# The last 64 channels of the centred rows transposed two tiles at a time in a fused convolution, Fourier and MLP kernel

## The reference

```python
batch, seq, d_model = (4, 4224, 192)          # H = 8 heads, K = 7 taps, rank 32, F = 768

# 1: causal depthwise convolution with softmaxed taps
x_unf = x_pad[:, idx, :].reshape(B, S, K, H, group)
x = np.einsum('hk,bskhg->bshg', w, x_unf).reshape(B, S, D)
# 2: low rank mixing over the sequence and the first MLP
u = x + ((x.transpose(0, 2, 1) @ U) @ V).transpose(0, 2, 1)
x = u + np.maximum(u @ w_ch1, 0.0) @ w_ch2
# 3: Fourier mixing over sequence and channels, normalisation, the second MLP
mixed = np.real(np.fft.fft(np.fft.fft(x, axis=1), axis=2))
u = x + mixed
mu = np.mean(u, axis=-1, keepdims=True)
var = np.mean((u - mu) ** 2, axis=-1, keepdims=True)
un = (u - mu) / np.sqrt(var + 1e-06)
out = u + np.maximum(un @ w2_ch1, 0.0) @ w2_ch2
```

## Time and profile before

| what | value |
|---|---|
| device time, median of 3 runs | 1253.76 us (1250.06 to 1254.5) |
| device time of the profiled execution | 1252.18 us |
| its span, first to last instruction | 1250.4 us |
| PE busy | 1218.8 us, 97% of the span |
| PEld busy | 1193.4 us, 95% |
| DVE busy | 821.1 us, 66% |
| ACT busy | 646.3 us, 52% |
| POOL busy | 425.8 us, 34% |
| mean granted clock of TensorE | 0.994 of full speed |

### The profile page before, as it was taken

How to read it: one execution, slowest core, us unless ns; L and a number is a source line. 1 busy time by engine, 2 the same in 40 slices (tenths; PEclk the granted TensorE clock), 3 DMA queues, 4 the chain that set the end, 5 groups by cost and what they waited for, 6 DMA issues and landing times.

```text
span 1250.4 us, 23662 instructions
## 1 busy us (share of the span) xinstructions
PE 1218.8 (97%) x8448; PEld 1193.4 (95%) x8448; DVE 821.1 (66%) x2191; ACT 646.3 (52%) x1603; POOL 425.8 (34%) x542
## 2 busy tenths in 40 slices
PE   6799999999999999999999999999999999999998
PEld 5699999999998999999999999999999999999998
DVE  4555576787765577655557777765666877766654
ACT  5355555444466555445555555544445555554553
POOL 0123352343344254333333244421212344533331
PEclk9899999999999999999999999999999999999999
DMA  8957553244556532224434322222323232322220
GB/s 283 279 185 232 178 160 91 85 147 141 163 168 216 196 123 90 74 69 135 136 96 138 115 92 87 92 70 81 95 86 106 85 101 92 92 93 86 86 68 29
DMA packets 87677, 154.46 MB, mean 124 GB/s; under 512 B 11448, under 2 KB 46627, under 8 KB 87516
## 3 DMA queue, kind: packets, MB, share of 16 engines
q1 hardware_dynamic: 79944, 133.95, 34.0%
q0 software_dynamic: 7616, 18.99, 4.7%
HBM read 94.59 MB, written 63.32 MB: 126 GB/s over the span
## 4 chain that ended last, share of the span: by engine, by line
PE 93%; DVE 2%; DMA 2%; issue 1%; POOL 1%; ACT 1%; SPq 0%; POOLq 0%; ACTq 0%
PE bank L802 20%; PE bank L803 9%; PE bank L783 8%; PE bank L790 7%; PE bank L791 7%; PE bank L787 7%; PE bank L784 7%; PE bank L839 4%; PE bank L806 4%; PE bank L892 4%; PE bank L855 2%; PE bank L915 2%; PE bank L857 2%; PE bank L856 2%; PE bank L876 2%; PE bank L805 2%
## 5 line engine op out<-in xcount | busy, mean ns | idle before, releaser
L987 ACT ACTIVATE ht<-bank 128x384 fp32r<-128x384 f32 x528 | 259.4, 491 | 506.8 <-PE bank L791 501.2
L1170 DVE SCALAR_TENSOR_TENSOR ht<-bank,ht 128x384 fp32r<-128x384 f32 x528 | 293.5, 556 | 339.6 <-ACT ht L987 332.6
L802 PE MATMUL bank<-w,ht 128*128 128x384 f32 x1320 | 418.6, 366 | 0.8 <-DVE ub L1178 0.5
L803 PE MATMUL bank<-w,ht 128*128 128x192 f32 x1320 | 331.0, 251 | 0.0
L1417 POOL TENSOR_TENSOR ub<-ub,tmp 128x576 f32<-128x576 f32 x88 | 126.0, 1432 | 462.5 <-DVE ub L1178 312.6
L802 PEld LDWEIGHTS bank<-w,ht 128*128 128x128 f32 x1320 | 248.8, 188 | 4.0 <-issue 3.1
L803 PEld LDWEIGHTS bank<-w,ht 128*128 128x128 f32 x1320 | 252.4, 191 | 0.0
L783 PE MATMUL bank<-uth,w1h 128*128 128x384 f32 x528 | 189.1, 358 | 0.0
L787 PE MATMUL bank<-utl,w1h 128*128 128x384 f32 x528 | 178.6, 338 | 0.3 <-DVE utl L1195 0.2
L790 PE MATMUL bank<-uts,w1s 128*128 128x384 f32 x528 | 178.5, 338 | 0.3
L784 PE MATMUL bank<-uth,w1l 128*128 128x384 f32 x528 | 178.2, 337 | 0.0
(11 more groups left out here) (118 smaller groups left out, 2218.8 us busy)
## 6 DMA issues: line engine op xcount, KB each, us to landing
f1t<-f_copy SPq DMA_DIRECT2D x44, 396.0 KB
ub<-x_two SPq DMA_DIRECT2D x44, 288.0 KB
mix<-mixed SPq DMA_DIRECT2D x44, 288.0 KB, 3.3
out<-ub SPq DMA_DIRECT2D x44, 288.0 KB
xin<-in_x SPq DMA_DIRECT2D x12, 864.0 KB, 6.9
x_conv<-xin SPq DMA_DIRECT2D x12, 756.0 KB
vch<-v_split SPq DMA_DIRECT2D x42, 192.0 KB
mixed<-rowk SPq DMA_DIRECT2D x88, 74.2 KB
```

What stands on the lines that cost most here:

```text
L802: e.matmul(dn[t][:, 0:2 * D], hh, w2[ph][:, m, :], start=(m == 0), stop=False)
L803: mm = e.matmul(dn[t][:, 0:D], hl, w2[ph][:, m, 0:D], start=False, stop=False)
L987: e.activation(hth[q % 4], up[q % 3][:, 0:TOK], ACT.Relu).then_inc(act_h, 1)
L1170: e.scalar_tensor_tensor(htl[q % 4], up[q % 3][:, 0:TOK], 0.0, hth[q % 4].bitcast(F32), ALU.max, ALU.subtract).then_inc(dve_l, 1)
```

## The change

In the second phase only, `un` is split into `un_first` (128 channels of each tile) and `un_rest` (the last 64 channels of the three tiles side by side, 192 columns). `centre` writes `un_first` in slot 4 with three activations of 128 columns, and a new `centre_rest` writes `un_rest` in slot 5 with three activations of 64 columns. `turn_centred` makes three transposes of `un_first`, one transpose of 128 columns of `un_rest` (tiles 0 and 1 together: their channels come out in partitions 0 to 63 and 64 to 127), and one of the last 64 columns (tile 2). ACT copies the second bank in two activations, DVE makes the low parts in two operations. For the middle tile the high part then lies in partitions 64 to 127 of `uts` and the low part in 0 to 63. The semaphore `act_un` counts six per block instead of three. The first phase is as it was.

```diff
-        un = sb("un", [128, TB, D], F32)
+        un_first = sb("un_first", [128, TB, 128], F32)
+        un_rest = sb("un_rest", [128, TB * 64], F32)
...
+        def outer_tiles(t, par, p0):
+            return t[p0:p0 + 64, par].rearrange("p (t q) -> p t q", t=TB)[:, 0::2, :]
...
+            def turn_centred(n):
+                k = count(n)
+                o, q = empty(e, ("turn", n, 0))
+                for t in range(TB):
+                    e.wait_ge(act_un, k * TB * 2 + t + 1)
+                    mm = e.transpose(o[:, t * 128:(t + 1) * 128], un_first[:, t, :], ident[:])
+                mm.then_inc(pe_tb[q], 1)
+                o, q = empty(e, ("turn", n, 1))
+                e.wait_ge(act_un, (k + 1) * TB * 2)
+                e.transpose(o[:, 0:128], un_rest[:, 0:128], ident[:])
+                e.transpose(o[0:64, 128:256], un_rest[:, 128:192], ident[:]).then_inc(pe_tb[q], 1)
...
-                copy(uts[0:64, par], o[0:64, 0:TOK]).then_inc(act_tb[q], 1)
+                if phase(n) == 0:
+                    copy(uts[0:64, par], o[0:64, 0:TOK]).then_inc(act_tb[q], 1)
+                else:
+                    copy(outer_tiles(uts, par, 0), o[0:64, 0:256].rearrange("p (t q) -> p t q", t=2))
+                    copy(uts[64:128, par, 128:256], o[64:128, 0:128]).then_inc(act_tb[q], 1)
...
-                    e.activation(un[:, t, :], u_slot(n)[:, t, :], ACT.Identity, bias=nm[:, n % 2, t:t + 1]).then_inc(act_un, 1)
+                    e.activation(un_first[:, t, :], u_slot(n)[:, t, 0:128], ACT.Identity, bias=nm[:, n % 2, t:t + 1])\
+                        .then_inc(act_un, 1)
+
+            def centre_rest(n):
+                for t in range(TB):
+                    e.activation(un_rest[:, t * 64:(t + 1) * 64], u_slot(n)[:, t, 128:D], ACT.Identity,
+                                 bias=nm[:, n % 2, t:t + 1]).then_inc(act_un, 1)
...
                     if m == 4 and ahead(n, 2) is not None:
                         deviation(n + 2)
                         centre(n + 2)
+                    if m == 5 and ahead(n, 2) is not None:
+                        centre_rest(n + 2)
...
-                e.tensor_tensor(uts[64:128, par], o[0:64, 0:TOK], uts[0:64, par].bitcast(F32), ALU.subtract)\
-                    .then_inc(tb_free[q], 1)
+                if phase(n) == 0:
+                    e.tensor_tensor(uts[64:128, par], o[0:64, 0:TOK], uts[0:64, par].bitcast(F32), ALU.subtract)\
+                        .then_inc(tb_free[q], 1)
+                else:
+                    e.tensor_tensor(outer_tiles(uts, par, 64), o[0:64, 0:256].rearrange("p (t q) -> p t q", t=2),
+                                    outer_tiles(uts, par, 0).bitcast(F32), ALU.subtract)
+                    e.tensor_tensor(uts[0:64, par, 128:256], o[64:128, 0:128], uts[64:128, par, 128:256].bitcast(F32),
+                                    ALU.subtract).then_inc(tb_free[q], 1)
```

More of the change, by code:

```diff
@@ L827, in turn @@
             def turn(n):
[L828 to L832, removed]
+                if phase(n) == 1:
+                    return turn_centred(n)
+                taken(e, ("low", n, 0))
+                taken(e, ("low", n, 1))
                 for half in range(2):
@@ L836, in turn @@
                     for t in range(TB):
-                        if ph == 1 and half == 0:
-                            e.wait_ge(act_un, k * TB + t + 1)
-                        mm = e.transpose(o[0:m, t * 128:(t + 1) * 128], src[:, t, c], ident[:])
+                        mm = e.transpose(o[0:m, t * 128:(t + 1) * 128], u_slot(n)[:, t, c], ident[:])
                     mm.then_inc(pe_tb[q], 1)
+            def turn_centred(n):
[9 more added lines that the diff above has]
+                e.transpose(o[0:64, 128:256], un_rest[:, 128:192], ident[:]).then_inc(pe_tb[q], 1)
             def dft128(n):
```

## The result

| | median us | runs | profiled execution us | its span us |
|---|---|---|---|---|
| before | 1252.96 (1250.06 to 1254.5) | 5 | 1252.18 | 1250.4 |
| changed | 1260.84 (1259.79 to 1261.95) | 5 | 1261.35 | 1259.4 |

The ratio of the times is 1.0062, with a 95% interval of 1.0050 to 1.0074: the changed kernel is 7.9 us slower. The forecast was 1257.4 us in a range of 1250 to 1263. So the sign was right, and the loss about twice the 3.6 us that were forecast.

A forecast was written before the change was run, and what follows sets the result against it. PE was taken to bound the kernel, with 93% of the chain. Terms -4.8 + 6.4 + 0.8 + 0.6 + 0.6 = +3.6 us gave a span of 1254.0 and a forecast median of 1257.4 us, range 1250 to 1263.

The forecast's parts named there:

- the transposes: PE at the turn: one step of 0.11 us goes per block, 44 x 0.11 = 4.8 us saved.
- The rival of whole transposes: At the turn on PE, the full 0.27 us is saved per block, 12.0 us instead of 4.8: 1250.2 us, chance 0.03.
- the twelve boundaries: Boundaries without groups or convolution: PE has no slack and waits 0.53 us at each, 12 x 0.53 = 6.4 us lost.
- The price of a piece: ACT at the block's end: 64-column activations cost 0.24 us each, three 0.72 us (bounds 0.57 and 1.04).
- the rival of dear pieces: Between L987 and L998 on ACT, three small pieces cost 0.35 us each: +8.9 us, 1262.7 us, chance 0.20.
- The cover at boundaries with groups: At the other 28 boundaries group_rows holds DVE or PE has more work: nothing lost, 0.3 us to spare with groups.
- the forecast's three terms for the 16 boundaries' waits: PE waits 0.53 us at twelve boundaries, 0.42 after blocks 42 and 64, 0.30 after 44 and 66: 6.4, 0.8, 0.6.
- blocks 44 and 66: First use of the turned rows there: PE already waits, so 0.14 us plus 0.15 for the split, 0.6 us for both.
- pure gain: At the block boundaries the pieces are absorbed and the transpose step goes: -4.8 us, 1249.0 us, chance 0.12.
- No price, except in blocks 44 and 66: Split copy and subtraction at the turn: 1.0 us of cover before uts' low part is read, so no cost elsewhere.
- under cover: Work behind partial on ACT (L987, some 0.3 us late) and on DVE is used two slots later, so costs nothing.
- the split's 0.15 us on DVE: At the turn, one more subtraction costs DVE 0.15 us fixed time; ACT's extra copy about as much.

The follow-up runs named there:

- the pieces alone: Kernel before with only the centre split, its three 64-column activations in slot 5, six transposes and single copies: 1261.42 us, ratio 1.0062.
- the pieces in slot 0 and the mean last: Changed kernel with centre_rest in slot 0 of the next block and DVE's aggregate and less_mean at the end of slot 2: 1246.54 us, ratio 0.9943.
- the pieces in slot 0: Changed kernel with centre_rest moved from slot 5 to slot 0 of the next block, behind hidden: 1251.77 us, ratio 0.9986.
- Moving the mean out of the way: DVE's aggregate and less_mean moved behind turned_low and x2_low: 1251.61 us in the changed kernel (single execution), 1250.44 us in the kernel before.

## Why the prediction was right, and where it fell short

**Right: the transposes.** One step of 0.11 us goes, not a length of 0.27: the turns without groups go from 11.16 to 11.04 or 11.05 us wherever the pieces are out of the way. The rival of whole transposes is out.

**Right: the twelve boundaries.** Their term was 12 x 0.53 - 12 x 0.11 = 5.0 us, and the stretch is 5.1 us longer. The price of a piece (0.24 us a step) was right too, so the rival of dear pieces is out although the time came near it; that was by another path. The cover at boundaries with groups held as well: with the pieces alone those blocks are as long as before, to 0.06 us. Between slot 5 and slot 0 the pieces cost 7.7 us by the stretches with six transposes (8.0 - 0.3) and 9.0 with five (7.05 + 1.96); the forecast's three terms for the 16 boundaries' waits were 6.4 + 0.8 + 0.6 = 7.8. Of these the 0.30 us after blocks 44 and 66 measured 0.23, and the 0.42 after blocks 42 and 64 0.47.

**Right: blocks 44 and 66**, the steps at the first use (0.29 us of 0.3), by the forecast's own working: with the pieces alone, where PE and the chain are late by the same, nothing is added there. **Right: pure gain is out**, at the places that the change chose; with the pieces in slot 0 and the mean last, most of it is there (3.8 us of 4.8).

**The step that failed** is "No price, except in blocks 44 and 66" for the split at the turn, together with the 44 x 0.11 that went before it and with the work behind `partial` that was to be "under cover". I read the cover of the turned rows, 1.0 us, at one block without groups and without `dft128`, and carried it to all. The stretches are 3.5 us longer than the forecast's terms, and the blocks say where:

- In blocks 26 to 31, 46, 47 and 68 to 74 `group_out` stands behind `turned_low` for its bank, and the 0.11 us are hardly gained: the turns go from 13.62 to 13.59, not to 13.51. That is 1.2 us.
- Blocks 22 and 23 together were to be 0.2 us shorter and are 0.5 longer: 0.7 us. The pieces have no part in it (0.03 us with them alone; 0.45 with them in slot 0).
- Blocks 45 and 67 were to be 0.30 - 0.11 = 0.2 us longer each and are 0.7: 1.0 us. With the pieces in slot 0 each is some 0.26 us longer: the 0.17 us of the pair are paid in full and the 0.11 not gained, since `dft128` waits for DVE's queue. With the pieces alone each is 0.5 longer: beside the boundary's 0.23, the late `add_residual` makes DVE's queue late for `dft128`, 0.27 us that the forecast had under cover.

The rest, some 0.5 us, lies for the most part in blocks 21, 24 and 25. Moving the mean out of the way confirms it: 3.0 us of the loss go (4.8 in the changed kernel, by a single execution, less 1.8 in the one before), and what is left of the change, 4.1 us, is near the 3.6 of the forecast's sum.

**Luck.** The time lies in the range of 1250 to 1263, but 0.3 us above the likeliest case's own range of 1255 to 1260.5, and the loss is twice the forecast's. That it is over 0.5% slower had a chance of 0.27, most of it for dear pieces, which did not come. No case of the forecast had the path that brought the second half of the loss; the width of the range took it in.

**A term that was mis-sized**: the split's 0.15 us on DVE. It is 0.17, and of that the part beyond 0.06 comes from lost overlap (last section). Alone it is small; where it lies on the path it counts with the waits behind it.

**What is not settled.** The stretches of kernels that differ in nothing that matters scatter by 0.2 to 0.4 us in sum, so the 0.5 us of blocks 21, 24, 25 and others has no cause of its own here. Of the 9.0 us by which the two spans differ, 1.8 lie in the first two blocks, which the change doesn't touch; in other kernels they came out between 1.4 us shorter and 2.0 longer. Blocks 24 and 25 differ from the kernel before by -0.4 to +0.3 us among the kernels, without a pattern; why is open.

## What to carry to other kernels

Before work is put between two instructions of an in-order engine, look at who waits for the second one: 0.72 us of small activations between a relu and a copy out of a bank cost 0.54 us at every boundary where PE had no slack, while the same work one slot later was free. Read the cover of an edit at every kind of block, not at the one whose timeline is easiest to read; a saved step on PE is worth little in blocks where PE's next wait ends on another engine, and work that is late in a queue has to be followed to everything that stands behind it. And when a change loses by its order, try its parts apart: here the merged transposes with the pieces in slot 0 and the mean last are 0.57% faster than before (0.38% to 0.75%), the quickest version of the study. The move of the mean has its share in that: alone, in the kernel before, it gives 0.17% (0.04% to 0.30%).

## What the runs showed of the hardware

**Overlap of neighbours.** Two subtractions of DVE in a row, 256 and 128 columns, follow each other by 0.342 us if they lie on the same 64 partitions, and by 0.431 if the second reads and writes the other half; in the other order the step is 0.306 us where the first lasts 0.293, so there too nothing overlaps. ACT's two copies step by 0.263 us on the same partitions and by 0.378 across (the first lasts 0.366). About 0.1 us of overlap is lost on both. Besides the partitions the change has a strided pattern for the outer tiles, and no experiment took one without the other. But the kernel before has pairs with plain patterns, the two copies and the two subtractions that fill `tst`. Each pair reads the same 32 partitions twice; ACT writes partitions 0 to 31 and then 64 to 95, DVE 32 to 63 and then 96 to 127:

```profile
444.71 0.73 ACT L977 ACTIVATE tst<-tsb 32x192 fp32r<-32x192 f32 x2
445.96 0.73 DVE L1318 TENSOR_TENSOR tst<-tsb,tst 32x192 fp32r<-32x192 f32 x2
```

ACT's second starts 0.370 us behind the first, which lasts 0.346, and DVE's 0.379 behind one of 0.348: no overlap, without a stride. The activations of `centre`, on the same partitions each time, do overlap (0.444 us long, 0.35 apart). So another set of partitions is enough to lose the overlap; whether a stride does it as well is not shown.

**TensorE's clock and block 32.** In block 32 PE stands idle for 1.62 us, in all twelve profiles of this study. Right behind it one execution runs at half the clock for 3.4 us and another doesn't. Columns: window us, length, then busy us of PE, PEld, DVE, ACT and POOL, granted clock, DMA share, GB/s. The kernel before:

```profile
518.60:520.60 2.00, 0.42 (x3) 0.25 (x3) 1.89 (x6) 0.49 (x1) 1.95 (x2) 1.00 0.25 72
520.70:524.10 3.40, 3.40 (x14) 3.40 (x15) 0.75 (x4) 0.25 (x1) 1.52 (x3) 0.53 0.30 108
```

and the kernel with pieces in slot 0 and the mean last:

```profile
521.70:525.10 3.40, 3.40 (x29) 3.39 (x29) 1.41 (x6) 1.12 (x4) 1.57 (x3) 1.00 0.31 110
```

The granted clock is 0.53 in the one, near the level of 1.2 GHz, and 1.00 in the other, and PE makes 14 matmuls where the other makes 29. Block 32 takes 18.0 us in the one case and 16.4 in the other. Six of the twelve profiles here have a stretch at half clock there (block 32 takes 18.0 us), among them before and changed; which kernels do follows no edit that I can see. It is 1.6 us of a difference that no comparison of single profiles should explain, which is why block 32 isn't in the table.
